# One fused attention, dense and expert kernel: ids loads behind the activations, a table in two parts, one ring of weight buffers

## The reference

```python
logits = x @ w_gate + modality_bias[modality_id]
e_idx = np.argmax(logits, axis=1)
...
for e in range(E):
    mask = e_idx == e
    h = np.maximum(x[mask] @ w1[e], 0.0)
    out[mask] = gate_w[mask, None] * (h @ w2[e])
```

## Time and profile before

| | us |
|---|---|
| median of 3 runs | 521.01 |
| lowest and highest | 519.86, 523.29 |
| profiled execution, own time | 520.04 |
| its span | 518.3 |
| PE busy in the span | 497.0 |
| DVE, ACT, POOL busy | 192.4, 181.1, 205.2 |

### The profile page before, as it was taken

The page is one execution under the profiler, slowest core; times in us unless marked ns, Lnnn a source line. Parts: engine busy times, 40 slices in busy tenths (PEclk is TensorE's granted clock), DMA queues, the critical chain, the costliest instruction groups (busy, mean ns, idle before and its releaser), DMA issues.

```text
span 518.3 us, 8805 instructions
## 1 busy us (share of the span) xinstructions
PE 497.0 (96%) x2974; PEld 403.8 (78%) x2975; DVE 192.4 (37%) x413; ACT 181.1 (35%) x309; POOL 205.2 (40%) x221
## 2 busy tenths in 40 slices
PE   7899999999999999999999999999897999999993
PEld 6778888888778888887888888887785888888850
DVE  4533332333334532222462366648211274222110
ACT  1233333334343444453443565521321282222210
POOL 2874654554315338443435755313120144111101
PEclk9999999999999999999999999999998999999997
DMA  6954434321020260001800000210372115888600
GB/s 205 405 225 162 164 123 155 132 96 35 0 82 1 83 242 0 0 0 73 332 1 1 2 0 0 76 64 24 103 271 72 41 41 201 256 279 263 196 1 20
DMA packets 24395, 57.36 MB, mean 111 GB/s; under 512 B 8247, under 2 KB 9919, under 8 KB 24368
## 3 DMA queue, kind: packets, MB, share of 16 engines
q1 hardware_dynamic: 18944, 50.23, 28.2%
q0 software_dynamic: 2544, 6.77, 3.9%
q10 hardware_dynamic: 2880, 0.02, 0.3%
HBM read 50.59 MB, written 6.61 MB: 110 GB/s over the span
## 4 chain that ended last, share of the span: by engine, by line
PE 88%; DVE 4%; DMA 3%; ACT 1%; issue 1%; ACTq 1%; POOL 0%; SPq 0%; POOLq 0%; DVEq 0%
PE psum L1381 9%; PE psum L1389 8%; PE psum L1391 8%; PE psum L1390 8%; PE psum L1383 8%; PE psum L1382 8%; PE psum L1470 4%; PE psum L1450 4%; PE psum L1472 4%; PE psum L1471 4%; PE psum L1452 4%; PE psum L1451 4%; PE psum L1344 2%; PE psum L1339 2%; PE psum L1322 2%; PE psum L1460 2%
## 5 line engine op out<-in xcount | busy, mean ns | idle before, releaser
L592 POOL TENSOR_TENSOR wi_lo<-wd_raw,wi_hi 128x512 fp32r<-128x512 f32 x48 | 62.1, 1294 | 145.0 <-ACT wi_hi L749 144.9
L1381 PE MATMUL psum<-xT,wi_lo 128*128 128x512 f32 x192 | 77.3, 402 | 0.0
L1389 PE MATMUL psum<-wo_hi,act_lo 128*128 128x512 f32 x192 | 75.7, 394 | 1.2 <-DVE act_lo L1009 1.2
L1383 PE MATMUL psum<-xT,wi_hi 128*128 128x512 f32 x192 | 75.0, 391 | 0.0
L1382 PE MATMUL psum<-xT,wi_hi 128*128 128x512 f32 x192 | 74.9, 390 | 0.0
L1391 PE MATMUL psum<-wo_hi,act_hi 128*128 128x512 f32 x192 | 74.8, 390 | 0.0
L1390 PE MATMUL psum<-wo_lo,act_hi 128*128 128x512 f32 x192 | 74.7, 389 | 0.0
L1006 DVE SCALAR_TENSOR_TENSOR act_f<-psum,act_f 128x512 f32<-128x512 f32 x48 | 33.1, 689 | 97.1 <-ACT act_f L767 96.6
L597 POOL TENSOR_TENSOR wo_lo<-wd_raw,wo_hi 128x512 fp32r<-128x512 f32 x48 | 61.9, 1289 | 2.7 <-ACT wo_hi L754 2.7
L767 ACT ACTIVATE act_f<-psum 128x512 f32<-128x512 f32 x48 | 28.6, 597 | 97.3 <-PE psum L1383 97.3
L1009 DVE TENSOR_TENSOR act_lo<-act_f,act_hi 128x512 fp32r<-128x512 f32 x48 | 33.8, 704 | 33.5 <-ACT act_hi L769 33.5
(11 more groups left out here) (203 smaller groups left out, 731.3 us busy)
## 6 DMA issues: line engine op xcount, KB each, us to landing
we_raw<-w_exp SPq DMA_DIRECT2D x48, 512.0 KB, 4.6
wd_raw<-w_dense SPq DMA_DIRECT2D x16, 512.0 KB, 5.6
qk_in<-attn_qk SPq DMA_DIRECT2D x10, 512.0 KB, 3.4
kv_in<-attn_kv SPq DMA_DIRECT2D x10, 512.0 KB, 3.4
x_d<-x_sb SPq DMA_DIRECT2D x12, 256.0 KB, 2.6
qk_more<-attn_qk SPq DMA_DIRECT2D x2, 512.0 KB, 6.8
kv_more<-attn_kv SPq DMA_DIRECT2D x2, 512.0 KB, 7.5
decay_mask<-pow_d SPq DMA_DIRECT2D x2, 256.0 KB, 4.0
```

The costliest lines, as they stand in the source:

```text
L592: nc.gpsimd.tensor_tensor(wi_lo[:, r, :], dense_raw(f, 0), wi_hi[:, r, :].bitcast(F32), ALU.subtract).then_inc(s_wil, 1)
L1381: nc.tensor.matmul(h, w_lo, hi, start=(c == 0), stop=False)
L1383: mm = nc.tensor.matmul(h, w_hi, hi, start=False, stop=(c == DC - 1))
L1389: nc.tensor.matmul(bank(ACC + i), lo, wo_hi[:, r, :], start=first, stop=False)
```

## The change

ScalarE's `load_ids(ids_n, t + 3)` moves behind `hid(t+1,0)` in the loop, behind the last splits in the `If` branch. Ahead of the loop, `relu(1,1)` and `rows(2)` move ahead of the wait for the table. On VectorE `evacuate_early(0)` and `hid(1,0)` move ahead of most of the table. The column of expert ids by place leaves `tab` (`val` has three columns, not four) and becomes part of `m_tab`, where the rests follow the whole experts in one list of 12 places; `loads` goes. SP has one loop over whole experts and rests, and a rest uses the buffer of its place modulo 3. TensorE waits for all weights once, on a register's value, ahead of `up_mixed(0)`.

```diff
@@ SP
             sp.wait_ge(s_tab, 1)
-            loads = sp.value_load(tab[0:1, LOADS_:LOADS_ + 1], min_val=RAWS, max_val=E)
             whole = sp.value_load(tab[0:1, WHOLE_:WHOLE_ + 1], min_val=KNOWN, max_val=E)
...
-            with sp.Fori(KNOWN, loads) as o:
-                e = sp.value_load(tab[0:1, bass.ds(ID_ + PRE + o, 1)], min_val=0, max_val=E - 1)
+            with sp.Fori(KNOWN, whole + MIX) as o:
+                e = sp.value_load(m_tab[0:1, bass.ds(o, 1)], min_val=0, max_val=E - 1)
...
-            for f in range(FC2):
-                sp.wait_ge(s_wer[f], 16 * loads)
-                sp.sem_inc(s_pass, 1)
-            sp.wait_ge(s_el, whole * FC2 + FC2)
...
-            for q in range(MIX):
-                e = sp.value_load(m_tab[0:1, q:q + 1], min_val=0, max_val=E - 1)
-                for f in range(FC2):
-                    if q * FC2 + f >= AHEAD:
-                        before_f = q * FC2 + f - AHEAD
-                        sp.wait_ge(s_mw[before_f % FC2], 16 * (before_f // FC2 + 1))
-                    sp.dma_start(we_raw[:, raw_mix(q), f, :], w_exp[bass.ds(e * FC2 + f, 1)].rearrange("a p n -> p (a n)")
-                                 ).then_inc(s_mw[f], 16)
@@ ACT
+            relu(1, 1)
+            rows(2)
             act.wait_ge(s_tab, 1)
             last = act.value_load(tab[0:1, LAST_:LAST_ + 1], min_val=PRE + MIN_TILES - 1, max_val=PRE + MAX_TILES - 1)
             load_ids(ids_n, PRE, s_ids)
-            relu(1, 1)
-            rows(2)
@@ ACT, If branch
                         split(k1, f, 0, raw)
-                    act.wait_ge(s_idc, t + 3)
-                    act.sem_inc(s_pass, 1)
-                    load_ids(ids_n, t + 3, s_ids)
                     hid(t, 1)
...
                         split(k1, f, 1, raw)
-                with act.Else():
                     act.wait_ge(s_idc, t + 3)
                     act.sem_inc(s_pass, 1)
                     load_ids(ids_n, t + 3, s_ids)
+                with act.Else():
                     hid(t, 1)
...
                     relu(t + 1, 0)
                     hid(t + 1, 0)
+                    act.wait_ge(s_idc, t + 3)
+                    act.sem_inc(s_pass, 1)
+                    load_ids(ids_n, t + 3, s_ids)
                 relu(t + 1, 1)
@@ DVE, table
-            tlink(nc.vector.tensor_tensor(tab_f[:, LOADS_:LOADS_ + 1], number[:, E - 1:E], live[:, E - 1:E], ALU.add))
-            nc.vector.tensor_copy(tab_f[:, WHOLE_:WHOLE_ + 1], tab_f[:, LOADS_:LOADS_ + 1]).then_inc(s_tb, 1)
...
-            nc.vector.tensor_scalar(tab_f[:, LOADS_:LOADS_ + 1], tab_f[:, LOADS_:LOADS_ + 1], float(RAWS), None, ALU.max)
+            nc.vector.tensor_tensor(tab_f[:, WHOLE_:WHOLE_ + 1], number[:, E - 1:E], live[:, E - 1:E], ALU.add)
...
             tlink(nc.vector.tensor_tensor(rel[:], t_iota[:], per_tile(pre), ALU.subtract))
-            nc.vector.tensor_tensor(place_eq[:], t_iota[:], per_tile(number), ALU.is_equal)
+            evacuate_early(0)
             nc.vector.scalar_tensor_tensor(out=val[:, 2], in0=rel[:], scalar=0.0, in1=per_tile(first_no[:]),
                                            op0=ALU.is_equal, op1=ALU.mult)
+            hid(1, 0)
             tlink(nc.vector.tensor_tensor(lt[:], rel[:], per_tile(n_til), ALU.is_lt))
-            nc.vector.tensor_tensor(val[:, 3], place_eq[:], per_tile(live_id[:]), ALU.mult)
...
-            evacuate_early(0)
-            hid(1, 0)
-            tlink(nc.vector.tensor_reduce(tab_f[:, 0:4 * NTAB], val[:].rearrange("p q t e -> p (q t) e"), AX_X, ALU.add))
+            tlink(nc.vector.tensor_reduce(tab_f[:, 0:3 * NTAB], val[:].rearrange("p q t e -> p (q t) e"), AX_X, ALU.add))
             nc.vector.tensor_copy(tab[:], tab_f[:]).then_inc(s_tab, 1)
@@ DVE, mixed table (in place of nine instructions)
+            places = t_iota[:, PRE:PRE + PLACES, :]
+            nc.vector.tensor_tensor(live_id[:], ord_id[:], live, ALU.mult)
+            nc.vector.tensor_tensor(m_id[:], ord_id[:], mixed[:], ALU.mult)
+            nc.vector.scalar_tensor_tensor(out=row_at[:], in0=n_til, scalar=float(P), in1=ord_slot[:], op0=ALU.mult, op1=ALU.add)
+            tlink(nc.vector.tensor_scalar(m_place[:], turn_no[:], tab_f[:, WHOLE_:WHOLE_ + 1], None, ALU.add))
+            nc.vector.scalar_tensor_tensor(out=row_at[:], in0=row_at[:], scalar=-float(SLOTS), in1=mixed[:], op0=ALU.add, op1=ALU.mult)
+            nc.vector.tensor_tensor(place_eq[:], places, per_place(number), ALU.is_equal)
+            tlink(nc.vector.tensor_tensor(m_eq[:], places, per_place(m_place[:]), ALU.is_equal))
+            nc.vector.tensor_tensor(m_val[:, 0], place_eq[:], per_place(live_id[:]), ALU.mult)
+            nc.vector.tensor_tensor(m_val[:, 1], m_eq[:], per_place(m_id[:]), ALU.mult)
+            tlink(nc.vector.tensor_tensor(m_val[:, 2], m_eq[:], per_place(row_at[:]), ALU.mult))
+            tlink(nc.vector.tensor_tensor(m_val[:, 0], m_val[:, 0], m_val[:, 1], ALU.add))
+            nc.vector.tensor_reduce(m_tab_f[:, 0:PLACES], m_val[:, 0], AX_X, ALU.add)
+            tlink(nc.vector.tensor_reduce(m_row[:], m_val[:, 2], AX_X, ALU.add))
+            tlink(nc.vector.tensor_reduce(m_tab_f[:, PLACES:], m_row[:].rearrange("p (k r) -> p r k", r=MIX), AX_X, ALU.add))
+            tlink(nc.vector.tensor_scalar(m_tab_f[:, PLACES:], m_tab_f[:, PLACES:], float(SLOTS), None, ALU.add))
             nc.vector.tensor_copy(m_tab[:], m_tab_f[:]).then_inc(s_mtab, 1)
@@ PE
             def up_mixed(q):
-                for f in range(FC2):
-                    pe.wait_ge(s_mw[f], 16 * (q + 1))
...
+            whole = pe.value_load(tab[0:1, WHOLE_:WHOLE_ + 1], min_val=KNOWN, max_val=E)
+            for f in range(FC2):
+                pe.wait_ge(s_wer[f], whole * 16 + 16 * MIX)
+                pe.sem_inc(s_pass, 1)
             pe.wait_ge(s_mx, 1)
             up_mixed(0)
```

More of the change, by code:

```diff
@@ L46 @@
 MX = MIX * MR
+PLACES = 4 * MIX
 PWW = 264
@@ L144, in fused_program @@
         spare = Placer(dense_off, dense_off + DENSE_W // 2)
-        rel, lt, inn, place_eq = (spare(name, [1, NTAB, E], F32) for name in ("rel", "lt", "inn", "place_eq"))
+        rel, lt, inn = (spare(name, [1, NTAB, E], F32) for name in ("rel", "lt", "inn"))
         cnt_by = spare("cnt_by", [1, E, E], F32)
         n_tri = spare("n_tri", [1, 2, E, E], F32)
-        val = spare("val", [1, 4, NTAB, E], F32)
+        val = spare("val", [1, 3, NTAB, E], F32)
         big = spare("big", [1, E], F32)
@@ L154, in fused_program @@
         rem_i = spare("rem_i", [1, E], I32)
-        at_mix = spare("at_mix", [1, MIX, E], F32)
         row_at = spare("row_at", [1, E], F32)
-        m_val = spare("m_val", [1, 2, MIX, E], F32)
+        m_place = spare("m_place", [1, E], F32)
+        m_id = spare("m_id", [1, E], F32)
+        place_eq = spare("place_eq", [1, PLACES, E], F32)
+        m_eq = spare("m_eq", [1, PLACES, E], F32)
+        m_val = spare("m_val", [1, 3, PLACES, E], F32)
+        m_row = spare("m_row", [1, PLACES], F32)
         place = Placer(dense_off, dense_off + DENSE_W)
@@ L204, in fused_program @@
         kept = sb("kept", [1, E], F32)
-        q_iota = sb("q_iota", [1, MIX, E], F32)
-        m_tab_f = sb("m_tab_f", [1, 2 * MIX], F32)
-        m_tab = sb("m_tab", [1, 2 * MIX], I32)
+        m_tab_f = sb("m_tab_f", [1, PLACES + MIX], F32)
+        m_tab = sb("m_tab", [1, PLACES + MIX], I32)
         ids_m = sb("ids_m", [P, 2], I32)
@@ L224, in fused_program @@
         pre_no = sb("pre_no", [1, 2, E], F32)
-        tab_f = sb("tab_f", [1, 4 * NTAB + 3], F32)
-        tab = sb("tab", [1, 4 * NTAB + 3], I32)
-        SB_, KT_, FI_, ID_, LAST_, LOADS_, WHOLE_ = 0, NTAB, 2 * NTAB, 3 * NTAB, 4 * NTAB, 4 * NTAB + 1, 4 * NTAB + 2
+        tab_f = sb("tab_f", [1, 3 * NTAB + 2], F32)
+        tab = sb("tab", [1, 3 * NTAB + 2], I32)
+        SB_, KT_, FI_, LAST_, WHOLE_ = 0, NTAB, 2 * NTAB, 3 * NTAB, 3 * NTAB + 1
         ids_pre = sb("ids_pre", [P, PRE, 2], I32)
@@ L345, in fused_program @@
         s_mgat = sem("mixed_rows_gathered")
-        s_mw = [sem(f"mixed_weights{f}") for f in range(FC2)]
         s_mt = sem("mixed_rows_transposed")
@@ L993, in _ @@
                 last = nc.vector.memset(tri[:, e, e:], 0.0)
-            for q in range(MIX):
-                last = nc.vector.memset(q_iota[:, q, :], float(q))
             last.then_inc(s_rt, 1)
@@ L1229, in _, with per_place @@
                                            op0=ALU.add, op1=ALU.add)
-            tlink(nc.vector.tensor_tensor(tab_f[:, LOADS_:LOADS_ + 1], number[:, E - 1:E], live[:, E - 1:E], ALU.add))
-            nc.vector.tensor_copy(tab_f[:, WHOLE_:WHOLE_ + 1], tab_f[:, LOADS_:LOADS_ + 1]).then_inc(s_tb, 1)
-            tb[0] += 1
-            dve.wait_ge(s_tb, tb[0])
-            nc.vector.tensor_scalar(tab_f[:, LOADS_:LOADS_ + 1], tab_f[:, LOADS_:LOADS_ + 1], float(RAWS), None, ALU.max)
+            nc.vector.tensor_tensor(tab_f[:, WHOLE_:WHOLE_ + 1], number[:, E - 1:E], live[:, E - 1:E], ALU.add)
```

(20 more changed lines are left out.)

9 lines of the change are left out of this document (1 added, 8 removed).

## The result

516.03 us in the median of 10 runs (513.87 to 518.41) against 521.52 of 10 runs before (519.56 to 525.28): 5.5 us, ratio 0.9886 with a 95% interval of 0.9856 to 0.9916. 514.3 had been forecast. The profiled execution took 516.76, span 515.0.

The account below looks back on a forecast made before the run. TensorE, 88% of the chain, was taken to bound the kernel, so only its stalls and slow stretches could be won. -4.9 - 1.6 + 0.3 + 0.2 = -6.0 from 520.04 gives 514.0, plus 0.3 for spread 514.3 us; range 511.8 to 518.3.

Parts of the forecast that it names:

- rival (a): Expert loop: the longer stream makes ids 4, 5 and 8 and their rows late, 2.2 not 0.3, 516.2 us; chance 0.20.
- -4.9 for the first loop tile: First loop tile: moving ids loads behind the activations removes the 3.0 us wait and slow stretch; bounds -4.9 and 0.
- -1.6 for the table: Before the loop: the new order turns three table waits, 2.34 us, into one up to 1.4; bounds -3.0 and 0.
- +0.2 for the tail: Ahead of `up_mixed(0)`: TensorE's register load and eight register waits cost 0.2 us, up to 1.1 if cover is short.
- +0.3 for gathers and ids beside the longer stream: At `transposes(5)`: ids 5 lose the old stall's cover, a stall of 0 to 1.1 us, taken as 0.3, stream traffic included.
- a wait for `xg` at tile 4: Expert loop: a TensorE wait for `xg` at tile 4, 5 or 8 would show the prediction wrong; no size given.
- the risk at tile 5: Tile 5, where ScalarE splits the next expert: tightest chain, rows in by 440.65, wanted 440.4; cost 0, upper end 0.3.
- rival (b): First loop tile: the stall stays, held elsewhere by `s_out` or `ids_s`, only the table's gain remains, 518.7 us; chance 0.08.
- (c): Expert loop: the stream makes gathers 5 and 6 over 3 us late, each costing 4.9, total 523.3 us; chance 0.05.
- (d): Before the loop: mixed table 1.6 us longer than summed, or its wait costs the clock; no gain there, 515.9; chance 0.10.
- Nothing on the path is won: Weight stream: the ring of buffers drops 4 MB of useless loads, 40 left, but gains no time on the path.
- The other signs: Expert stage: no wait over 1.5 us, first loop tile 12.3 at clock 1.00, one `xe_lo` wait about 1.4, 40 loads.

Follow-up runs that it names:

- ids_behind: Kernel before with only the ids loads moved behind the activations, in both branches: 516.07 us, ratio 0.9932.
- old_ids_order: Changed kernel with the ids loads back ahead of `hid(t,1)`, leaving the new table and the ring: 520.99 us, ratio 1.0005.
- table_order: Kernel before with only the order ahead of the loop changed, both tables as they were: 519.76 us, ratio 0.9996.
- Lo_first: Changed kernel with `rows_lo(2)` on VectorE ahead of the mixed table, directly behind the cast of the table: 515.46 us, ratio 0.9874.
- the third profile: Changed kernel measured a third time, nothing altered: 515.19 us, ratio 0.9883; 153.15 us from transposes of tile 2 to end of span.
- the first profile: Changed kernel as first measured: 516.03 us, ratio 0.9886; 156.35 us from transposes of tile 2 to end of span.
- the second: Profile of the changed kernel measured again, nothing altered: 516.69 us, ratio 0.9940; 154.01 us from transposes of tile 2 to end of span.
- orders_only: Kernel before with both changes of order, neither the new table nor the ring: 515.37 us, ratio 0.9912.
- lo_first_no_ring: Kernel before with both changes of order and `rows_lo(2)` ahead of its mixed table, no new table, no ring: 513.60 us, ratio 0.9856.
- thin_rests: Changed kernel with the last two rests loaded thin, 32 of 1024 columns of each slice: 514.74 us, ratio 0.9897.
- lo_first_one: Changed kernel with `rows_lo(2)` ahead of the mixed table and one slice in flight, not two: 512.80 us, ratio 0.9842.

## Why the prediction was right, point by point

The forecast of 514.3 was 1.7 us low, inside its range of 511.8 to 518.3; the way was right. Of the 1.7 us, 0.5 is the kernel before, whose median was 521.52 in this measurement and 521.01 in the one the forecast started from; the gain was 5.5 us where 6.7 had been forecast. 516.03 lies nearer to rival (a), 516.2, than to the forecast. By its terms:

- **-4.9 for the first loop tile**: -4.85 in the table, and alone 4.62 of stage (ids_behind). Right, with the mechanism: undone by itself, it takes the whole gain back, also that of the order ahead of the loop (old_ids_order, table_order). How much it is in the mean of many runs is less certain than the two profiles make it look: 1.9 of the 4.9 us were the slow clock of one execution, and such a stretch did not follow the longer wait of old_ids_order; the ratio of ids_behind says 3.5 us.
- **-1.6 for the table**: -1.63, all of it by the order; the old table in the new order gave 1.9. The steps hold nearly one by one. `down(1,0)` followed the transposes with no wait; `m_tab`'s cast ended at 362.96 (362.75 forecast); and `rows_lo(2)` came directly behind it:

```profile
362.80 0.16 DVE L1248 CAST m_tab<-m_tab_f 1x15 int32<-1x15 f32 x1
362.89 0.67 DVE L1072 TENSOR_TENSOR xe_lo<-psum,xe_hi 128x512 fp32r<-128x512 f32 x1
```

  Lo_first shows that this order was the whole of the leftover wait.
- **+0.2 for the tail**: 0. (Its upper price of 1.1 us needs a part of the cover: 17 steps at 0.05 to 0.1 us alone are 0.9 to 1.7 us.) From transposes 9 to `up_mixed(0)` it was 42.26 us before (495.29 - 453.03) and 42.25 after:

```profile
492.14 3.66 PE L1587 MATMUL psum<-we_raw,xT_m 128*32 128x256 f32 x64
```

- **+0.3 for gathers and ids beside the longer stream**: the term that was mis-sized. Against the third profile, whose loop is free of waits, it measured 3.2 us in the first and 0.9 in the second, and a wait for `xg` at tile 4, which the prediction named as a sign of being wrong, came in both. Two sub-steps failed. First, I put the risk at tile 5, whose chain I summed to the edge; gather 5 was in time in all three, and the one that was late was gather 4, which stood beside the old stream too, and which I had priced only in rival (a). In the first profile its ids took 4.3 us and its gather 6.3, above the maximum of 5.7 that bounded my sum. The kernel before had left it little room: issued at 380.9, it landed after 4.7 us, 0.6 us ahead of the transposes at 386.21. Second, I followed `ids_n` through all tiles and costed the later ones at nothing, which was right, and did not follow `ids_s` and the scatters. They stand in rival (b) as something that might hold tile 3. They did make the scale of tile 3 late (`ids_s` 6.3 us), without a wait of TensorE, and then those of tiles 4 and 6, and with them `he_lo` of the tiles behind, by the loop from scatter to `s_out` to `ids_s` to the scale of y; 1.67 us between transposes 5 and 9.
- Rival (a) has about the right price (516.2), in part by luck. Of its three places only gather 4 was late (1.51 us, priced at 0.8); its largest, tile 5 at 1.1, and tile 8 were not, and the larger half of the loss, the `ids_s` loop, is not in it. (c) and (d) did not come.
- "Nothing on the path is won" by the ring: right (orders_only, lo_first_no_ring).
- The other signs that it named held: no wait over 1.5 us, a first loop tile of 12.37 us at granted clock 1.00, one wait of 1.16 us for `xe_lo`, 40 loads of `we_raw`, the last issued at 436.3.

What is shown: the place of the loads makes most of the gain, the order ahead of the loop 1.6 to 1.9 us of it, and the slices moved beside the loop make `ids_s` land later. What is argued: that this traffic is what costs time. The profiles fit it (four of the five with the ring and two slices in flight have new waits, the four variants without the ring and thin_rests have none in the loop apart from the old one, or one of 0.3 us), but the unchanged kernel also ran once without any. What made gather 4 late in some executions stays open, and so does the size of the loss in the mean of many runs. The medians of the changed kernel differ by 1.5 us from set to set, so 0 to 3.2 us from three profiles is all that can be said.

## What to carry to other kernels

Put a small load that waits on another engine behind the activations of its tile, not ahead of them, and follow every small transfer of the tile, the scatter's ids and the scatter's own landing as well as the gather's, with the landing times that they have beside the bulk stream to come, not the one of before. If bulk loads have slack (here the weights were wanted 50 us later), take depth from them first: one slice in flight was fast enough, and the loads of ids landed sooner beside it. And when a chain on an in-order engine gets longer, ask which short instruction stands behind it; here moving one instruction ahead of 16 shortened its stretch by 1.4 us.

## What the runs showed of the hardware that was not expected

A 1 KB load (`ids_s`) that lands in 1.7 us alone took up to 6.3 us with two 512 KB slices in flight (6.8 in lo_first), up to 4.2 with one (in lo_first_one), and 2.3 in thin_rests. The Trainium skill, DMA: Bandwidth & Descriptors, section "Issuing engines are not separate DMA queues", says that transfers of all issuing engines interleave on the same 16 DMA engines, and these times agree in kind. The fixed cost of about 2 us in the Trainium skill's "Anatomy of one DMA" (same page), given there for DMAs that GpSimd issues, does not hold for this load of ScalarE beside such a stream.

The granted clock did not follow the length of a wait alone. The 3.0 us of the earlier trace rows was followed by a stretch at 0.57, a wait of 3.8 us in table_order by one at 0.56; but the 3.44 us of old_ids_order was not, and neither was the 1.36 us at 386.25 (granted clock 1.00 from 386.0 to 398.6). Windows of table_order behind its wait, and of old_ids_order ahead of and behind its own:

```profile
396.20:400.00 3.80, 3.76 (x10) 2.95 (x11) 0.00 (x0) 0.55 (x1) 0.00 (x0) 0.56 0.23 63
```

```profile
393.50:397.07 3.57, 0.13 (x2) 0.01 (x1) 0.69 (x1) 0.68 (x2) 1.18 (x2) 1.00 0.53 182
397.07:400.50 3.43, 3.43 (x17) 2.88 (x18) 0.00 (x0) 0.51 (x1) 0.00 (x0) 1.00 0.88 287
```

So the 1.9 us that the clock added to the old wait need not be there in every execution of the kernel before, which could be one more source of its spread; only one execution of it was profiled, so this is not shown.
